# A routed expert tile of 192 slots: 128, and 64 held beside their low halves, with two weight streams instead of three

## What is computed

```python
def _moe2_ref(x, w_skip, w_gate, w1, w2):
    do_compute = x @ w_skip > 0
    out = x.copy()
    xc = x[do_compute]
    logits = xc @ w_gate
    e_idx = np.argmax(logits, axis=1)
    # probs: softmax of logits; gate_w: the chosen expert's share
    y = np.zeros_like(xc)
    for e in range(E):
        mask = e_idx == e
        h = np.maximum(xc[mask] @ w1[e], 0.0)
        y[mask] = gate_w[mask, None] * (h @ w2[e])
    out[do_compute] = xc + y
    return out
```

## Time and profile before

| what | us |
|---|---|
| time, median of 3 runs (lowest, highest) | 728.56 (727.1, 730.04) |
| the profiled execution's own time | 726.63 |
| its span, first to last instruction | 725.0 |
| TensorE busy | 682.8 |
| VectorE, ScalarE, GpSimd busy | 394.2, 367.8, 158.4 |
| attention and dense layer, tile 0's first half | until 545 |
| expert tiles on TensorE | 545 to 707.6 |
| from the last matmul to the end | 17.4 |

### The profile page before, as it was taken

One profiled execution on the slowest core, in us unless ns is written; L12 is line 12 of the kernel. 1 busy time (PEld: TensorE's weight loads), 2 busy tenths in 40 slices (PEclk: granted clock), 3 DMA queues, 4 the chain that ended last, 5 costly groups with the idle time before them and its releaser, 6 DMA issues.

```text
span 725.0 us, 14342 instructions
## 1 busy us (share of the span) xinstructions
PE 682.8 (94%) x4569; PEld 591.7 (82%) x4570; DVE 394.2 (54%) x1363; ACT 367.8 (51%) x1034; POOL 158.4 (22%) x206
## 2 busy tenths in 40 slices
PE   4889999999999999999999999999988899999990
PEld 3578888888888899999999999889866688887870
DVE  5867665555565343343343433345565866567674
ACT  5788766556565333323333333344435865557671
POOL 5345322222231010010010100100223433213431
PEclk9999999999999999999999999999999999999996
DMA  7648534223321422002001020013117885647861
GB/s 258 199 141 259 189 112 146 72 73 129 101 87 40 151 69 77 12 1 88 1 28 61 0 87 0 0 61 86 45 61 246 282 262 183 212 151 248 257 189 59
DMA packets 48216, 85.60 MB, mean 118 GB/s; under 512 B 7619, under 2 KB 11715, under 8 KB 48161
## 3 DMA queue, kind: packets, MB, share of 16 engines
q1 hardware_dynamic: 43664, 79.20, 33.5%
q0 software_dynamic: 3952, 4.65, 2.2%
q10 hardware_dynamic: 544, 1.05, 0.4%
HBM read 70.84 MB, written 18.52 MB: 123 GB/s over the span
## 4 chain that ended last, share of the span: by engine, by line
PE 85%; issue 5%; DVE 3%; ACT 2%; DMA 2%; POOL 2%; POOLq 1%; SPq 0%; DVEq 0%; ACTq 0%
PE ph L1324 28%; PE px L1337 28%; PE pe_h L1420 7%; PE py L1446 7%; PE pscore L1274 3%; PE pctx L1296 3%; PE ptrans L1283 3%; PE ph L1354 2%; PE phT L1432 1%; ACT w_hi L759 1%; PE ph L1348 1%; DMA w_raw<-wf 1%; PE pxT L1400 1%; POOL probs L638 1%; DMA xg<-x_dram,gather_slots 1%
## 5 line engine op out<-in xcount | busy, mean ns | idle before, releaser
L1324 PE MATMUL ph<-x_hi,w_hi 128*128 128x256 f32 x576 | 166.8, 290 | 1.2 <-DVE x_lo L992 1.2
L1087 DVE SCALAR_TENSOR_TENSOR gated<-gated,ph 128x256 f32<-128x256 f32 x144 | 60.7, 421 | 195.6 <-ACT gated L829 194.1
L1324 PE MATMUL ph<-x_hi,w_lo 128*128 128x256 f32 x576 | 162.7, 283 | 0.0
L1324 PE MATMUL ph<-x_lo,w_hi 128*128 128x256 f32 x576 | 162.4, 282 | 0.0
L829 ACT ACTIVATE gated<-ph 128x256 f32<-128x256 f32 x144 | 55.1, 383 | 128.1 <-PE ph L1324 128.1
L1337 PE MATMUL px<-w_hi,g_hi 128*128 128x512 f32 x288 | 117.7, 409 | 0.0
L1337 PE MATMUL px<-w_hi,g_lo 128*128 128x512 f32 x288 | 113.5, 394 | 0.0
L1324 PEld LDWEIGHTS ph<-x_hi,w_hi 128*128 128x128 f32 x576 | 108.7, 189 | 5.7 <-DVE x_lo L992 1.5
L1337 PE MATMUL px<-w_lo,g_hi 128*128 128x512 f32 x288 | 113.3, 393 | 0.0
L1324 PEld LDWEIGHTS ph<-x_lo,w_hi 128*128 128x128 f32 x576 | 108.6, 189 | 4.0
L1324 PEld LDWEIGHTS ph<-x_hi,w_lo 128*128 128x128 f32 x576 | 108.5, 188 | 0.0
(11 more groups left out here) (193 smaller groups left out, 1116.3 us busy)
## 6 DMA issues: line engine op xcount, KB each, us to landing
w_raw<-we SPq DMA_DIRECT2D x72, 256.0 KB
more_raw<-we SPq DMA_DIRECT2D x72, 256.0 KB
w_raw<-wf SPq DMA_DIRECT2D x32, 256.0 KB
vs<-vw SPq DMA_DIRECT2D x16, 384.0 KB, 3.2
qs<-qT SPq DMA_DIRECT2D x16, 288.0 KB, 3.4
ks<-kT SPq DMA_DIRECT2D x16, 288.0 KB, 4.2
xT_dram<-x_stage SPq DMA_DIRECT2D x16, 288.0 KB, 2.9
x_lo<-xT_dram SPq DMA_DIRECT2D x8, 512.0 KB, 3.9
```

The source lines that it names most:

```text
L1087: nc.vector.scalar_tensor_tensor(gated[s % 2][:, :], gated[s % 2][:, :], 1.0, ph[s % 2][:, 0:TT], ALU.add, ALU.mult).then_inc(gated_done, 1)
L1324: last = nc.tensor.matmul(ph[f % 2][:, 0:TT], up_w(w, k, f), x[p][:, k, :], start=(at == 0 and n == 0), stop=(at == KD - 1 and n == 2))
```

## The change

A tile has 192 slots: 128 in the first part, and 64 in the second (`REST`). The second part's operand holds 128 columns: the high parts of the 64 tokens, and beside them their low parts (`xe_rest`, `h_rest`). One matmul with high weights then gives high by high and low by high at once, in rows 0-63 and 64-127 of the accumulator, and one with low weights the rest (low by low too). So a block takes two matmuls instead of three. The two groups of rows have to be added: for h before the relu, by a VectorE reduce from the transposed bank (`sum_h`, new), after which ScalarE takes relu and high part from `h_sum` (SBUF) and VectorE the low part; for the output by a third row operation. ScalarE's `relu` of the second part is a plain copy. The first part is computed as before. The token transposes are made by part, not by pairs of k; `e_up` of a part waits for that part's low half. The number of tiles is counted by comparison and sum instead of a shift, the lists of `meta` grow from 18 to 22 places, and the tile loops from 16 to 20.

Its core (tables, names and the gather's shapes left out):

```diff
             def split_h_hi(t, h, o):
...
+                if h == 0:
+                    act.wait_ge(h_transposed, (t * EH + h) * EFO + o + 1)
+                    nc.scalar.activation(h_hi[:, at, :], phT[o][:, :, :], ACT.Copy).then_inc(h_hi_done, 1)
+                else:
+                    act.wait_ge(h_summed, t * EFO + o + 1)
+                    nc.scalar.activation(h_rest[:, at, 0, :], h_sum[:, at, :], ACT.Relu).then_inc(h_hi_done, 1)
...
+            def sum_h(t, o):
+                at = slice(o * FPO, (o + 1) * FPO)
+                dve.wait_ge(h_transposed, (t * EH + 1) * EFO + o + 1)
+                wait(dve, h_hi_done, ((t - 1) * EH + 1) * EFO + o + 1)
+                wait(dve, h_lo_done, ((t - 1) * EH + 1) * EFO + o + 1)
+                nc.vector.tensor_reduce(h_sum[:, at, :], phT[o][:, :, :].rearrange("p f (a t) -> p f t a", t=REST),
+                                        AX.X, ALU.add).then_inc(h_summed, 1)
 
             def split_h_lo(t, h, o):
...
+                else:
+                    dve.wait_ge(h_summed, t * EFO + o + 1)
+                    nc.vector.scalar_tensor_tensor(h_rest[:, at, 1, :], h_sum[:, at, :], 0.0, h_rest[:, at, 0, :].bitcast(F32),
+                                                   ALU.max, ALU.subtract).then_inc(h_lo_done, 1)
...
-                    add_rows(1).then_inc(rows_done[p], 1)
+                    dve.wait_ge(e_down_done, t * EH + 2)
+                    add_rows(1).then_inc(rest_rows_begun, 1)
+                    dve.wait_ge(rest_rows_begun, t + 1)
+                    add_rows(1, REST, rows).then_inc(rows_done[p], 1)
 
                 if is_first(t):
                     next_lo(0, 1, 2)
-                    split_h_lo(t, 1, 0)
-                    split_h_lo(t, 1, 1)
+                    for o in range(EFO):
+                        sum_h(t, o)
+                        split_h_lo(t, 1, o)
...
                     next_lo(3, 4, 5)
+                    sum_h(t, 0)
+                    next_lo(6)
                     split_h_lo(t, 1, 0)
-                    next_lo(6, 7, 8)
+                    next_lo(7, 8)
                     xe_split_lo(t + 1, 1 - p)
+                    sum_h(t, 1)
                     split_h_lo(t, 1, 1)
...
+                    else:
+                        for n, w in enumerate((w_hi, w_lo)):
+                            last = nc.tensor.matmul(pe_h[o][:, :], xe_rest[p][:, k, :, :], e_up_w(w, p, k, o),
+                                                    start=(k == 0 and n == 0), stop=(k == KD - 1 and n == 1))
...
+                    else:
+                        for n, w in enumerate((w_hi, w_lo)):
+                            last = nc.tensor.matmul(py[h][:, :], h_rest[:, f, :, :], e_down_w(w, p, f),
+                                                    start=(f == 0 and n == 0), stop=(f == EFB - 1 and n == 1))
```

More of the change, by code:

```diff
@@ L53 @@
 EFB = EF // P
-ET = 256
-EH = ET // P
+ET, EH = 192, 2
+REST = ET - P
 EFO = EF // CH
@@ L280, in plist_in @@
         def plist_in(bank):
-            return bank[:, 0, 0:1]
+            return bank[0:REST, 0, 0:1]
         ffn.close()
@@ L1393, in tile, with transpose_part @@
                         down(t - 1, FB - 1)
+            def transpose_part(p, h):
+                n = part(h)
+                for k in range(KD):
+                    last = nc.tensor.transpose(xe_bank(h)[:, k, :], xg[p][0:n, h, k * P:(k + 1) * P], ident[0:n, 0:n])
+                last.then_inc(xe_transposed, 1)
             def transpose_xe(t, p, uses):
                 pe.wait_ge(gathered[p], (uses + 1) * 16 * EH)
[L1397 to L1403 removed]
+                wait(pe, xe_lo_done, t * EH)
+                for h in range(EH):
+                    transpose_part(p, h)
             def h_bank_free(t, h, o):
@@ L1487, in first_transposes @@
                 pe.wait_ge(gathered[0], (h + 1) * 16)
-                for k in range(KD):
-                    last = nc.tensor.transpose(first_pxT(h)[:, k, :], xg[0][:, h, k * P:(k + 1) * P], ident[:, :])
-                last.then_inc(xe_transposed, 1)
+                transpose_part(0, h)
             def list_late():
```

154 lines of the change are left out of this document (75 added, 79 removed).

## The result

The changed kernel takes 724.69 us (median of 9 runs, 722.71 to 728.13), the kernel before beside it 729.39 (9 runs, 726.68 to 732.07). The ratio is 0.9945, interval 0.9922 to 0.9967: **4.0 us less, 2.4 to 5.7**, where 7.3 were forecast. (The medians alone differ by 4.7; gains of whole kernels are by the ratio throughout.) The predicted time of 721.2 is 3.5 too low, and the measured one lies inside the stated range of 715 to 726; the median before came out 0.8 above the one the forecast started from.

A forecast was written before the change was run, and what follows sets the result against it. TensorE was taken to bound the full expert tiles. The terms, -1.6 - 10.5 + 0.2 + 2.0 + 2.6, gave -7.3 us, hence 721.2 us in the median, with a range of 715 to 726 (-4 to -10, chance 0.62).

The forecast's parts named there:

- Term 1: Full expert tiles: fewer second-half matmuls on TensorE save 3.73 us each, 18.7 us over five, as the ceiling.
- Term 2: End of full tiles: TensorE waits 1.1 us for h's low parts, leaving -2.6 us each in tiles 2, 3, 4, 6.
- Term 3: Tile 0: a weight chunk's fixed arrival holds the relu, so -1.6 us instead of -3.7; longer lists cost 0.
- Term 4: Short tiles: the sum's longer VectorE and ScalarE chain delays the next tile, +2.0 us after tile 5, +0.2 for tile 1.
- Term 5: The tail, tile 7: VectorE's longer chain to the row operations costs +2.6 us; the third row operation is hidden.
- Hides behind the first scatter: In the tail, the third row operation (0.7 to 0.8 us) costs nothing, as the first scatter holds GpSimd until the second.
- uncovered 0.8: In the tail, the third row operation's cost if the first scatter did not hide it: 0.8 us.
- The clock: Rival: TensorE's clock falls from 2.4 to 1.2 GHz after short tile 5; +11 us, 740; chance 0.02.
- a clock below 1.00: Sign that the forecast is wrong: TensorE's granted clock under 1.00.
- One sign: Sign of being right: tile 7's last row operation about 21.5 us after its start instead of 18.9.
- Less is kept: Rival: later buffer reloads make the second bank's relu late by 1 us in six tiles; -1.3 us, 727.3; chance 0.16.
- More is kept: Rival: small operations overlap better, removing full-tile waits and part of the short tile's 2.0; 715.5 to 717 us; chance 0.15.

The follow-up runs named there:

- second profile of after: The changed kernel, unchanged, run and profiled a second time; 723.48 us (7 runs), ratio 0.9934 to the kernel before.
- short_lists: The changed kernel with room for 16 tiles instead of 20, so shorter lists and two loop passes less; 721.01 us, ratio 0.9888.
- late_split: The changed kernel, with VectorE waiting before a tile's last two weight chunks until GpSimd has issued the first scatter; 723.22 us, ratio 0.9928.
- Filler: The changed kernel with next-tile weight chunks 6 and 7 rounded before the first bank's sum, second bank's order kept; 721.51 us, ratio 0.9895.
- reorder: The changed kernel with chunks 6 and 7 ahead of the first sum's rounding and the second sum ahead of xe low; 716.04 us, ratio 0.9831.

## Why the prediction gave too large a gain

Its direction and most of its waits were right, its sum was not. Step by step, against the second profile of after:

- **Term 1** right: 80 matmuls gone. As to duration 3.73 holds in before's layout.
- **Term 2** right in mechanism: wait 0.89 (1.1 forecast), sum 0.68 (0.69). Yet the full tile is 22.6, not 22.4. The wait's 0.89 is from end to start; from start to start it costs 1.04, and the matmul behind it another 0.1. The rest, 0.12, is the start of the down matmuls after the token transposes: 0.91 behind the first of them in after, 0.79 in before, though four are narrower. Over four tiles **+0.8** of the miss.
- **Term 3** near (-1.8 for -1.6, with a fall of the clock inside); its claim that the lists cost 0 was wrong by **+0.3** (short_lists).
- **Term 4** right for tile 5 (+1.8). For tile 1 the +0.2 came out at +0.9 (**+0.7**). This profile has a fall of the clock there, behind an idle stretch of 1.14 us, but late_split has tile 1 at 17.87, the same +0.7, with none. Filler and reorder, with another order and no fall there, have 17.34 and 17.36, the +0.2 of the forecast. So the clock isn't needed for it; which wait makes it stays open.
- **Term 5** right up to the row operations (+2.4). "Hides behind the first scatter" is **the step that failed in kind**: the scatter has no fixed end behind which something could hide. It ends 0.94 us after the two weight chunks that follow the row operations on VectorE, and the third row operation pushes these back by 0.75. The "uncovered 0.8" was the true price, **+0.7**: rows to end went from 13.17 to 13.90, and to 13.26 without the operation.
- **The clock** had 0.02, and "a clock below 1.00" stood among the signs of being wrong. It did fall, for 3 to 7 us at a time and not for a whole tile. In after's first profile falls, late weights and late rows together cost 6 us.

The misses add up to 2.5 against gains of 0.5 not forecast (tiles 0, 5 and 7): -7.3 becomes -5.3. From there to the -4.0 and -4.8 measured is 0.5 to 1.3, within the intervals. The later start (538.8 in the mean against 537.5 and 538.2), clock, late weights and late rows are what the record has for it, not shown in size. The median minus the profile, which the forecast carried over as 1.9, is 2.8 in before's nine runs. One sign was misread: from tile 7's first matmul to its first row operation before takes 19.08, not 18.9.

"Less is kept" named late reloads and a late relu. TensorE did wait longer for the relu, 2.60 us in tile 0 of the first profile and 1.14 in tile 1 of the second (0.25 and 0.59 in before's first profile, 0.66 and 0.95 in its second); behind the first stood a late first load, not a reload. "More is kept" asked for overlap of the small operations; it takes the other order, and then it comes in full.

## What to carry to other kernels

When a chain crosses two engines several times, the order of the two queues decides what the change is worth: the same operations, interleaved, gave 12 us instead of 4 to 5. Before calling an operation hidden behind a DMA that GpSimd issues, look whether VectorE's next operations read two operands from SBUF; here the DMA's issue then ended with them, and a late one of them was paid in full. An experiment that shortens a list also moves all that lies behind it: hold addresses fixed, or test them alone. And before a profile without falls of the clock is called typical, its mean clock is to be held against those of the other executions.

## What the hardware showed that was not expected

- The same matmuls, 24 in a row, took 5.57 to 5.61 us or 5.45 to 5.46 depending on where the tiles of tokens and h lie in SBUF (640 bytes per partition apart), with the weights unmoved and the clock at 1.00. A full tile gained 0.3 us. Which bits of the address matter wasn't tried.
- The granted clock fell to 0.50 for 3 to 7 us at a time in ten of eleven profiles with the new tile, in the first profile of after behind 2.60 and 1.18 us and behind 2.58 us without a matmul. One and the same stretch of 2.07 to 2.43 us had a fall behind it in eight of eleven, and one of 2.50 and 2.46 in neither profile of before. With idle matmuls cut to fit these stretches it stayed at 1.00 in four of four; with longer ones that left two such stretches open it fell in two of two.
- The first scatter of a tile, issued by GpSimd, ended 0.91 to 0.95 us after VectorE's run of two-operand operations if these began before it (1.88, 1.91 or 3.17 us long), and also if they began 0.48 after it while a row operation ran (2.70). It took 1.05 to 1.08 if they began 0.13 (before) or 0.91 after it, or not beside it at all.
